# Router logits: four 32-column TensorE tiles summed afterwards, or one accumulated matmul of nine columns

## The reference

```
logits = np.einsum('bsd,de->bse', x, w_gate)                 # 512 -> 8 experts
local_gate = 1.0 / (1.0 + np.exp(-np.einsum('bsd,de->bse', x, w_local).squeeze(-1)))
for b in range(B):
    for s in range(S):
        fresh_e = int(np.argmax(logits[b, s]))
        e = fresh_e if s == 0 or local_gate[b, s] < 0.5 else prev_e
        p = softmax(logits[b, s])
        out[b, s] = p[e] * (np.maximum(x[b, s] @ w1[e], 0.0) @ w2[e])
```

## Time and profile before

| | us |
|---|---|
| median of 3 runs | 701.06 |
| lowest and highest | 697.13, 701.18 |
| the profiled execution's own time | 701.06 |
| its span in the profile | 699.3 |
| outside the span | 1.8 |

### The profile page before, as it was taken

One profiled execution on the slowest core, in us unless ns is written; L12 is line 12 of the kernel. 1 busy time (PEld: TensorE's weight loads), 2 busy tenths in 40 slices (PEclk: granted clock), 3 DMA queues, 4 the chain that ended last, 5 costly groups with the idle time before them and its releaser, 6 DMA issues.

```text
span 699.3 us, 14070 instructions
## 1 busy us (share of the span) xinstructions
PE 628.7 (90%) x4645; PEld 507.8 (73%) x4645; DVE 508.9 (73%) x993; ACT 354.8 (51%) x560; POOL 203.8 (29%) x161
## 2 busy tenths in 40 slices
PE   3888888898359999999999999985699999999997
PEld 3566666675337888888888888873588888888886
DVE  2555555566649899889989988981779777787772
ACT  2455655552047877878787777872232232322321
POOL 2000000025335546456554655433712011000000
PEclk9999999999569999999999999997799999999999
DMA  8846455418841107174416254402211020100102
GB/s 280 254 146 206 155 198 168 160 56 298 335 155 32 46 30 285 45 285 163 161 51 219 96 191 134 155 24 77 57 41 46 2 90 30 55 5 0 60 1 75
DMA packets 37946, 85.06 MB, mean 122 GB/s; under 512 B 7825, under 2 KB 8977, under 8 KB 37905
## 3 DMA queue, kind: packets, MB, share of 16 engines
q1 hardware_dynamic: 29776, 61.44, 25.4%
q0 software_dynamic: 4960, 17.30, 7.5%
q10 hardware_dynamic: 3168, 5.77, 2.2%
HBM read 69.30 MB, written 15.20 MB: 121 GB/s over the span
## 4 chain that ended last, share of the span: by engine, by line
PE 87%; DVE 6%; issue 2%; DMA 2%; POOL 1%; SPq 1%; ACT 1%; POOLq 0%; DVEq 0%; ACTq 0%
PE ps L839 21%; PE ps L841 21%; PE ps L840 21%; PE ps L690 3%; PE ps L660 3%; PE ps L870 3%; PE ps L686 3%; PE ps L627 2%; PE ps L663 2%; PE ps L848 1%; DVE y_g L1262 1%; DVE l_p L1013 1%; PE ps L923 1%; PE ps L628 1%; DMA b_x<-x_rows,block_i 1%
## 5 line engine op out<-in xcount | busy, mean ns | idle before, releaser
L1416 ACT CAST w_h<-slots 128x1024 fp32r x88 | 92.0, 1048 | 50.2 <-PE ps L841 28.3
L1422 ACT CAST w_h<-slots 128x1024 fp32r x88 | 89.5, 1050 | 39.5 <-PE ps L841 25.2
L1218 DVE TENSOR_TENSOR w_l<-slots,w_h 128x1024 fp32r<-128x1024 f32 x66 | 87.4, 1372 | 11.8 <-ACT w_h L1416 9.1
L1225 DVE TENSOR_TENSOR w_l<-slots,w_h 128x1024 fp32r<-128x1024 f32 x66 | 77.9, 1233 | 15.8 <-ACT w_h L1422 15.8
L1496 ACT ACTIVATE h_buf<-ps 128x512 f32<-128x512 f32 x32 | 19.2, 601 | 123.3 <-PE ps L841 108.2
L527 POOL TENSOR_TENSOR w_l<-slots,w_h 128x1024 fp32r<-128x1024 f32 x22 | 54.1, 2460 | 77.4 <-ACT w_h L1416 77.4
L839 PE MATMUL ps<-w_h,b_hTh 128*128 128x512 f32 x176 | 71.6, 407 | 2.6 <-DVE b_hTl L1212 2.6
L839 PE MATMUL ps<-w_h,b_xTh 128*128 128x512 f32 x176 | 71.2, 404 | 1.6 <-DVE b_xTl L1205 1.6
L841 PE MATMUL ps<-w_h,b_xTl 128*128 128x512 f32 x176 | 69.6, 395 | 0.0
L840 PE MATMUL ps<-w_l,b_xTh 128*128 128x512 f32 x176 | 69.5, 395 | 0.0
L841 PE MATMUL ps<-w_h,b_hTl 128*128 128x512 f32 x176 | 69.4, 394 | 0.0
(11 more groups left out here) (224 smaller groups left out, 1416.2 us busy)
## 6 DMA issues: line engine op xcount, KB each, us to landing
slots<-w SPq DMA_DIRECT2D x16, 2048.0 KB, 12.8
l_va<-va SPq DMA_DIRECT2D x16, 520.0 KB, 4.1
l_k<-kw SPq DMA_DIRECT2D x16, 352.0 KB, 3.3
y_sorted<-b_y ACTq DMA_DIRECT2D x22, 256.0 KB, 2.6
l_q<-ql SPq DMA_DIRECT2D x16, 256.0 KB, 3.4
x_rows<-X POOLq DMA_DIRECT2D x4, 1024.0 KB, 5.4
out<-o_l SPq DMA_DIRECT2D x4, 1024.0 KB, 4.2
win<-w_in POOLq DMA_DIRECT2D x1, 2048.0 KB, 11.5
```

What stands on the lines that cost most here:

```text
L1218: vec.tensor_tensor(w_l[:, u, :], unit_of(at, False, u), w_h[:, u, :].bitcast(F32), ALU.subtract).then_inc(w_lo_dve, 1)
L1225: vec.tensor_tensor(w_l[:, u, :], unit_of(at, True, u), w_h[:, u, :].bitcast(F32), ALU.subtract).then_inc(w_lo_dve, 1)
L1416: sca.copy(w_h[:, u, :], unit_of(at, False, u)).then_inc(w_hi, 1)
L1422: sca.copy(w_h[:, u, :], unit_of(at, True, u)).then_inc(w_hi, 1)
```

## The change

The four chunks' matmuls of `logits` now write the same nine partitions, as one accumulated product (start on the first chunk, stop on the last). gate_w has nine columns a chunk and no zero columns, r_lT has nine partitions, and `copy_logits` copies nine partitions. `turn_logits` no longer sums: it is a transpose of a 9x128 piece of r_lT, with a 9x9 identity as the moving operand. The constant C_SUM goes, so that the constants have 1249 columns instead of 1258. The order of the instructions and their waits on each engine stay as they are; the buffers behind the constants lie 384 bytes lower.

```
-C_SUM = C_ROW + 1
-C_MASK = C_SUM + E + 1
+C_MASK = C_ROW + 1
...
-        gate_w = place("const", "gate_w", [P, DC, 32])
+        gate_w = place("const", "gate_w", [P, DC, E + 1])
...
-        r_lT = place("route", "r_lT", [P, TILES * P])
+        r_lT = place("route", "r_lT", [E + 1, TILES * P])
...
                 for c in range(DC):
-                    last = mm(ps[32 * c:32 * c + 32, 6 + g % 2, 0:n], gate_w[:, c, :], r_xT[g % 2][:, c, 0:n],
-                              start=True, stop=True)
+                    last = mm(ps[0:E + 1, 6 + g % 2, 0:n], gate_w[:, c, :], r_xT[g % 2][:, c, 0:n],
+                              start=(c == 0), stop=(c == DC - 1))
                 last.then_inc(lt_ready, 1)
 
             def turn_logits(g):
                 pe.wait_ge(lt_copied, g + 1)
                 for tile in tiles_of[g]:
-                    last = mm(ps[:, 5, (E + 1) * tile:(E + 1) * (tile + 1)], r_lT[:, P * tile:P * tile + P],
-                              consts[:, C_SUM:C_SUM + E + 1], start=True, stop=True)
+                    last = nc.tensor.transpose(ps[:, 5, (E + 1) * tile:(E + 1) * (tile + 1)],
+                                               r_lT[:, P * tile:P * tile + P], consts[0:E + 1, C_ID:C_ID + E + 1])
                 return last
...
-                vec.tensor_copy(r_lT[:, P * tiles_of[g][0]:P * tiles_of[g][0] + n], ps[:, 6 + g % 2, 0:n]
+                vec.tensor_copy(r_lT[:, P * tiles_of[g][0]:P * tiles_of[g][0] + n], ps[0:E + 1, 6 + g % 2, 0:n]
                                 ).then_inc(lt_copied, 1)
...
-    for chunk in range(DC):
-        c[32 * chunk:32 * chunk + E + 1, C_SUM:C_SUM + E + 1] = np.eye(E + 1)
...
-    gates = np.concatenate([inputs["moe_w_gate"], inputs["moe_w_local"], np.zeros((DM, 32 - E - 1), np.float32)], axis=1)
+    gates = np.concatenate([inputs["moe_w_gate"], inputs["moe_w_local"]], axis=1)
...
-        "wg": np.ascontiguousarray(gates.reshape(DC, P, 32).transpose(1, 0, 2)),
+        "wg": np.ascontiguousarray(gates.reshape(DC, P, E + 1).transpose(1, 0, 2)),
```

## The result

| | kernel before | changed |
|---|---|---|
| median, us | 697.25 (20 runs) | 703.62 (20 runs) |
| lowest and highest, us | 694.96, 701.18 | 699.06, 708.65 |
| ratio, 95% interval | | 1.0088 (1.0068 to 1.0108) |
| span of the profiled execution, us | 699.3 | 703.2 |

The change makes the kernel slower by 0.88%, 6.1 us (4.7 to 7.5). The predicted change was +5.6 us, the predicted time 706.7 us. The forecast stood on 701.06 us, the median of three runs that were on the high side of the 20. The two spans differ by less, 3.9 us. That difference is of little use as a whole, because attention, which the change does not touch, ran 2.8 us shorter in the profiled execution of after: routing's transposes start at 152.26 us instead of 155.04 us. In the profiles of this study that start lies anywhere from 149.99 to 155.04 us.

The account below looks back on a forecast made before the run. TensorE was taken to bound routing, with the first gather next on the chain. Stage 11.0 - 2.1 + 0.3 - 0.1 = +9.1 us, less 3.5 at the gather, gave +5.6 on 701.06: 706.7 us, range 703.5 to 711.0.

Parts of the forecast that it names:

- Logits, +11.0 us: Routing's logits groups: chunks follow one another, eight passes instead of two, 10.4 us for four groups and 0.65 us for GT.
- rival B: Logits groups: weight loads of up to 0.11 us show between passes, 3.9 us more, net +9.5, 710.6 us; chance 0.12.
- The turn, -2.1 us: Routing's summing step becomes a transpose, one record a tile instead of two, so half of 4.20 us goes; bounds 0 to -2.3.
- Rival F: Routing's turn: the nine-row transpose takes two records, net +7.7 us, 708.8 us; chance 0.07.
- Entering, leaving and cover, +0.2 us: Routing: lost overlap at shape changes +0.3 us, transposes of X waiting less for copies -0.1, GT's copy cover 0 to 0.1.
- The gather, -3.5 us: First block's row gather: issued after expert 2's weights end, it needs 3.4 us instead of 6.97, giving 3.5 us back.
- Rival C: First gather: its 7 us are a first-time cost, so nothing is given back; net +9.1, 710.2 us; chance 0.08.
- Rival D: Routing's logits stage: the clock falls, half of 32 long passes run at 1.2 GHz, 6.9 us more, 713.6 us; chance 0.08.
- The rest of the kernel follows the first block with its loads and all: Everything behind the first gather's landing: one constant shift, no further gain or loss, 0 us.
- rival E: First block and convolution start: clock stays up, 5.3 us would go, 701.4 us, not measurably slower; chance 0.05.
- A's range: The forecast itself, whole kernel: +5.6 us, 3.5 to 7.5 with the terms' bounds and about a microsecond for the clock; chance 0.60.
- the shifted buffers have no row that gives them a price: Buffers behind the smaller constants: their shift was entered at 0 us.

Follow-up runs that it names:

- the hold: Kernel before, expert 2's weights issued only when the first two gathers have landed: ratio 0.9934; the same edit on the changed kernel: 1.0106.
- twice: Kernel before with each logits group's matmuls issued a second time: ratio 1.0005 to the kernel before.
- pad: Changed kernel with 384 unused bytes behind the constants, so large buffers lie where they lay before: ratio 1.0130 to the kernel before.
- two_pass: Changed kernel with the turn as an ordinary fp32 matmul with the 9x9 identity instead of a transpose: 706.52 us, run once.
- packed logits: Kernel before with each of a group's four tiles accumulating its four chunks in its own 32 array columns: ratio 1.0010, with expert 2's weights held back 0.9942.
- warming: Kernel before, expert 2's weights held back, plus constant matmuls on TensorE around the first block's row transposes: ratio 0.9949 with eleven, 0.9922 with sixteen.
- its repeat: Changed kernel run again unaltered for more runs, against the kernel before: ratio 1.0110, 7.7 us slower.

## Why the prediction was right up to the first block, and wrong behind it and in its call

**What bounds the stage**: right. Every piece of it is TensorE's in both kernels.

**Logits, +11.0 us**: 4 x 3.53 + 0.97 = 15.09 us against 4.33, +10.8. The pass of 0.433 us was worked out from two widths and held; the weight loads are hidden (rival B is refuted).

**The turn, -2.1 us**: 4 x 0.34 + 0.24 = 1.60 us against 4.20, -2.6. The step took the price of a pass over to a transpose; a transpose of nine rows costs 0.085 us, below the bound that I drew from the transposes of X. Rival F is refuted by 17 records.

**Entering, leaving and cover, +0.2 us**: the transposes of X take 6.36 us instead of 6.16, and 0.03 us of the last copy shows, since the four turns that cover it take 0.34 us and not the 0.50 of the prediction. Stage: 10.8 - 2.6 + 0.2 = +8.4 us; +9.1 was forecast, and 8.2 to 10 was its range.

**The gather, -3.5 us**: right, 6.97 to 3.44 us, and its reason is shown by the hold (3.43 us in the old kernel) and by twice. Rival C is refuted. Rival D did not come: the logits groups stay at the passes of the fast clock.

**"The rest of the kernel follows the first block with its loads and all", 0 us**: this step failed. It is +1.8 us in the traces of the pair, and 501.2 to 502.2 us in all four traces of the changed kernel and its variants with hold or pad (500.0 in two_pass), against 499.3 to 501.2 in five traces with the old or packed logits and no warming. Some 1.0 us of it are the clock, 0.55 in the experts' stage and 0.49 at the start of the convolution. I had both places as rival E, but only as a gain, and "about a microsecond" in A's range without a sign. It was a loss, and a repeated one, because the rise came late against the work. The other 0.8 us are the term that I put at 0 for want of a row, "the shifted buffers have no row that gives them a price": the pad takes it away again in the trace. That the whole came out only 0.5 us above the forecast is in part luck, since the stage came out 0.7 us below its term and the part behind it 1.8 us above.

**The base**: "The profiled execution has the median's time, so the sum holds against both" used three runs. The 20 runs have a median 3.8 us lower, and so the time came out at 703.62 us, at the range's lower edge, while the change was 0.5 us larger than forecast.

**The call**: 0.61 went to within 1%. The measured +0.88% lies there, and its repeat +1.10% beyond it, but neither is no change: 20 runs a side give 0.2% of uncertainty. The forecast of +5.6 us, with a range of changes of +2.4 to +9.9 us that left zero out, said slower. "Within 1% (7 us) is about what a measurement of this kernel tells from no change" was the sentence that turned a slower kernel into a likely sameness.

## What to carry to other kernels

Work moved on the critical engine is paid in full only up to the next transfer on the chain: look which traffic that transfer shares the DMA queues with, whether that traffic moves along, and hold it back if nobody needs it yet. Narrow outputs with a long contraction are cheap beside one another on different columns of the array and dear one after another; if different rows take the columns, the sum comes for free as well. After a pause of TensorE count the clock's return as a term with two signs, since it does not keep step with the work. And price a shift of the buffers, however small: here 384 bytes were worth 0.7 to 0.8 us in a stage that the change does not touch.

## What the runs showed of the hardware

An fp32 matmul with 9 columns of weights costs the same per pass as one with 32, 0.43 us for 512 columns. Four of them on different columns of the array take 1.00 us together and on the same columns, one after the other, 3.53 us. A turn of 9x128 by transpose costs 0.085 us a tile and by fp32 matmul 0.12 us a pass, 0.98 us for four tiles with nine rows as with 128 (0.99 us). An indirect gather of 128 rows lands after 3.4 to 3.6 us on idle or nearly idle queues and after 7.0 to 7.8 us while 2 x 2048 KB of another queue are under way. And the clock, once up, fell again at the start of the first block after TensorE had been idle twice, for 0.68 and 1.57 us; with the second gap filled by five matmuls it stayed. The same matmuls of the convolution stage, at 2.4 GHz, took 190.7 us with the buffers 384 bytes lower and 190.0 us without.
